# Moving an attention kernel's operands as two parts of 48 rows instead of one of 104

## The chip, the core and the metric

The kernel runs on one core of a Trainium2 chip. The core has five engines with queues of their own: TensorE (PE, with its weight loads as PEld), VectorE (DVE), ScalarE (ACT), GpSimd (POOL) and SyncE (SP), which here issues all transfers and does nothing else. The core's 16 DMA engines carry the transfers. The metric is the device time of one execution in microseconds; a run's result is the median of its executions.

## The reference

Three stages follow each other: a recurrence over 768 steps for 4 x 8 heads of 40 dimensions, a two-layer MLP (320 to 2048 to 320, 3072 tokens) and a mixture of four two-layer experts (320 to 1024 to 320).

```python
for t in range(S):                                    # r, k, v, w, a, b: [4, 8, 768, 40]
    y[:, :, t] = einsum('bhd,bhde->bhe', rt, state)
    Sa = einsum('bhde,bhe->bhd', state, at)
    state = state * wt - outer(Sa, bt) + outer(vt, kt)
x = y as [3072, 320]
x = (h - tanh(h)) @ w_out             with h = x @ w_in
out = sum over e of p[:, e] * (relu(x @ w1[e]) @ w2[e])
```

## The kernel before, in words

**The work.** The 768 steps are cut into 6 chunks of 128. A *unit* is one chunk of a group of four heads (48 units, `i`), and two units make a *pair* (24 pairs, `p`; four pairs make a chunk). Each pair runs on PE as a chain of four blocks of 32 steps, in which PE, DVE and ACT hand small tiles to each other (`right_sides`, `save_right_side`, `answer`, `save_answer`). After the last pair of each chunk from the second on, one pass of the first MLP runs for the chunk before (`mlp`). The experts follow, in a part of the program of their own.

**The operands.** Two heads stand above each other in one tile: rows 0 to 39 and rows 64 to 103. Rows 40 to 63 hold nothing but padding. So every operand tile has 104 rows (`PR = HALF + HD`, 64 + 40). For each unit SP loads raw decays, k, b and a (`raw_parts`, L220) into one of seven buffers at the start and later into one of five and then three (`slot`). DVE scans the decays (L1045) and takes the reciprocal (L1051), POOL scales k and b (L1241) and a (L1244) in place, PE makes the unit's diagonal blocks (`diagonal`, L583), and SP stores the scaled operands to HBM (`store_operands`, L369). For each pair SP later loads them back by pairs of units: k and b (`load_kb`, L379), a (`load_a`, L388) and the decays (`load_decays`, L397).

**The order.** SP's list is written out by hand (`start`, `early_loads`, `pair`, `mlp` of the SP block) and runs strictly in order; each step waits on semaphores for the buffer it writes. A later raw load waits for the store of the unit that had its buffer. During pairs 2 to 7 the same list also brings the first MLP's weights in eight pieces (`raw_piece`, L453: L469, L471 twice, L472), and during pair 5 the first tokens (L449, L451); ACT rounds them (L947 to L949 and L956), POOL takes the rest (L1261 to L1267). ACT does this in line with its other work for the pairs.

**The start.** The loads of the first seven units stand in a program block of their own. All engines leave that block together, when SP has issued the last of its 21 transfers; DVE's first scan comes behind it. From there DVE works through eight units, two masks, two more units and the inverse of the first chunk (L1070 to L1092) before PE can start on pair 0.

Of the kernel before, what the change touches and what calls it, by code (L numbers as in the profile page):

```python
# [26 lines left out]
C = 128  # L27
# [8 lines left out]
HALF = 64  # L36
# [38 lines left out]
def uses(i):  # L75

    return sum(slot(k) == slot(i) for k in range(i + 1))
# [85 lines left out]
def recurrence_and_first_mlp(nc, sem, pairs, ident, kbaw, rvt, vn, w_in, w_out, scratch, turned, middle):  # L163
    ctx = ExitStack()
    with ctx:
# [195 lines left out]
        def _(sp):  # L361
            def load_raw(i):
                j = before(i)
                if j is not None:
                    sp.wait_ge(op_stored[slot(j)], 16 * uses(j))
                    sp.wait_ge(lt_full, j + 1)
                raw_parts(sp, i)

            def store_operands(i):  # L369
                sp.wait_ge(scaled, 2 * (i + 1))  # L370
                sp.dma_start(scratch[i, :, :], raw_of(i)[0:PR, WW:MADE]).then_inc(op_stored[slot(i)], 16)

            def both_units(p):

                for i in (2 * p, 2 * p + 1):
                    sp.wait_ge(op_stored[slot(i)], 16 * uses(i))
                return scratch[2 * p:2 * p + 2, :, :].rearrange("j p w -> p j w")

            def load_kb(p):  # L379

                both = both_units(p)
                if p >= 2:
                    sp.wait_ge(kbn_full[1], p - 1)
                    sp.wait_ge(low_full, p - 1)
                sp.dma_start(kb[:, p % 2, :, :, :, :].rearrange("p j a q t -> p j (a q t)"), both[:, :, 0:OP_A])\
                    .then_inc(kb_in[p % 2], 16)

            def load_a(p):  # L388
# [5 lines left out]
                a = at[:, p % 2, :, :, :].rearrange("p j q t -> p j (q t)")  # L394
                sp.dma_start(a, both[:, :, OP_A:OP_LAM]).then_inc(at_in[p % 2], 16)

            def load_decays(p):  # L397

                both = both_units(p)
                if p >= 2:  # L400
                    sp.wait_ge(y_saved, p - 1)
                    sp.wait_ge(state_ready, p - 1)
                sp.dma_start(lam[:, p % 2, :, :, :].rearrange("p j q t -> p j (q t)"), both[:, :, OP_LAM:OPW])\
                    .then_inc(lam_in[p % 2], 16)

# [47 lines left out]
            def raw_piece(i):  # L453
# [4 lines left out]
                if not earlier:  # L458
                    last = LAST_RAW[piece_slot(i)]
                    sp.wait_ge(op_stored[slot(last)], 16 * uses(last))  # L460
# [108 lines left out]
        def _(pe):  # L569
# [155 lines left out]
            def scores(p, j):  # L725

                if j == 0:
                    pe.wait_ge(kb_in[p % 2], 16 * (p // 2 + 1))
                    pe.wait_ge(at_in[p % 2], 16 * (p // 2 + 1))
                    pe.wait_ge(r_in[p % 3], 64 * (p // 3 + 1))  # L730
# [171 lines left out]
        def _(act):  # L902
# [19 lines left out]
            def save_turned_answers(p):  # L922
                act.wait_ge(ut_full, p + 1)
                if p == 0:
                    act.wait_ge(op_stored[RING + 1], 16)
                act.activation(ut[:, :, :, :].rearrange("p j q t -> p (j q) t"),
                               turn_bank[0:PR, 0:4 * C].rearrange("p (k t) -> p k t", k=4), ACT.Copy).then_inc(ut_saved, 1)
# [108 lines left out]
        def _(dve):  # L1036
# [21 lines left out]
            def inverse(c, first, last):  # L1058
# [4 lines left out]
                for k in range(first, last):  # L1063
                    if k == 0:
# [3 lines left out]
                        elif c:  # L1068
                            dve.wait_ge(op_stored[RING + 1], 16)
                        ins = dve.transpose(lu[:, :, :], ld[:, :, :].rearrange("p h t -> p t h"))  # L1070
# [50 lines left out]
            def mask_ur(p):  # L1121
                dve.wait_ge(ur_full, p + 1)
                if p == 0:
                    dve.wait_ge(op_stored[RING], 16)
                dve.tensor_tensor(out=nu[:, :, :, :, :].rearrange("p s j q t -> p s (j q) t"),
# [13 lines left out]
            def save_result(p):  # L1139
                dve.wait_ge(y_full, p + 1)  # L1140
                dve.wait_ge(lam_in[p % 2], 16 * (p // 2 + 1))
                if p:
# [94 lines left out]
        def _(pool):  # L1237
# [9 lines left out]
            def decay_state(p):  # L1247
                g = 2 * (p % PPC)
                pool.wait_ge(st_read, p + 1)
                pool.wait_ge(lam_in[p % 2], 16 * (p // 2 + 1))  # L1250
                both = st[:, g:g + 2, :, :].rearrange("p j q e -> p (j q) e")
# [307 lines left out]
```

## Time and profile before

| | before |
|---|---|
| median of 3 runs | 1663.45 us (1659.49 to 1669.53) |
| the profiled execution | 1664.84 us, span 1663.1 us |
| PE busy | 1484.1 us, 89% |
| DVE, ACT, POOL busy | 811.2, 420.4, 374.4 us |
| mean granted TensorE clock | 0.953 |
| moved by DMA | 112.84 MB |

The span runs from the first to the last instruction; some 1.7 us of the execution lie around it. Busy time is what an engine spends in instructions; idle time is given to what ended it. Only idle time on the chain that ends last costs anything. SP's rows show how long the issue of a transfer occupied SP's sequencer, not how long the transfer took. The share of DMA is a mean over all 16 engines.

### The profile page before, as it was taken

To read this page: it belongs to the slowest core of one execution; us is meant where nothing else is said; L and a number is where in the kernel's file an instruction comes from. 1 tells how busy PE (TensorE), PEld (TensorE's weight loads), DVE (VectorE), ACT (ScalarE), POOL (GpSimd) and SP (SyncE) were. 2 spreads that over 40 slices of the span, in tenths; PEclk is the share of its full clock that TensorE was granted. 3 is DMA by queue.
4 is the path that set the end of the run, shared out by engine and by line. 5 is a ranking of instruction groups with operands and counts; after the bars stand their busy time and mean duration, and the time that the engine had idled before them with its cause. 6 is when DMAs were issued, how large, how long until landed. Compare 5 with 4: busy or idle time off the path is not lost. (4 is left out here: it accounts for less than half of the span.)

```text
span 1663.1 us, 37883 instructions
## 1 busy us (share of the span) xinstructions
PE 1484.1 (89%) x15888; PEld 1295.1 (78%) x15888; DVE 811.2 (49%) x1396; ACT 420.4 (25%) x859; POOL 374.4 (23%) x314
## 2 busy tenths in 40 slices
PE   2387688998989999999969779999999999999998
PEld 1266566877877877877868679999999999999998
DVE  7959765776865955853211323333333333333333
ACT  1123343343333233333223311111111111111111
POOL 4122553332332322321233340202020202020000
PEclk9978798999998988998989889999999999999999
DMA  6545684065066135111010420101010100000011
GB/s 183 163 129 144 161 216 109 17 179 145 11 161 159 31 109 133 37 56 41 9 35 1 147 70 0 35 0 35 0 35 0 34 0 18 17 0 0 0 47 47
DMA packets 89411, 112.84 MB, mean 68 GB/s; under 512 B 10952, under 2 KB 67400, under 8 KB 89288
## 3 DMA queue, kind: packets, MB, share of 16 engines
q1 hardware_dynamic: 89288, 111.05, 24.2%
q8 instruction: 96, 1.57, 0.4%
q14 instruction: 27, 0.22, 0.0%
HBM read 78.73 MB, written 32.28 MB: 67 GB/s over the span
## 5 line engine op out<-in xcount | busy, mean ns | idle before, releaser
L1443 PE MATMUL banks<-x2t,u 128*128 x1536 | 377.6, 393 | 8.4 <-POOL u L1410 8.4
L1453 PE MATMUL banks<-u,hid 128*128 128x320 f32 x2304 | 360.6, 309 | 0.0
L1453 PEld LDWEIGHTS banks<-u,hid 128*128 128x128 f32 x2304 | 349.0, 188 | 11.2
L1508 DVE SCALAR_TENSOR_TENSOR hid<-banks,hid 128x512 fp32r<-128x512 f32 x192 | 132.7, 691 | 414.0 <-ACT hid L1478 414.0
L1443 PEld LDWEIGHTS banks<-x2t,u 128*128 128x128 f32 x1536 | 284.2, 189 | 61.3 <-issue 8.6
L1478 ACT ACTIVATE hid<-banks 128x512 fp32r<-128x512 f32 x192 | 115.0, 599 | 581.5 <-PE banks L1443 581.5
L859 PE MATMUL banks<-xt,wi 128*128 128x512 f32 x768 | 197.6, 400 | 20.5 <-issue 12.8
L868 PE MATMUL banks<-wo,hid 128*128 128x320 f32 x1152 | 183.8, 309 | 5.6 <-POOL hid L1283 5.6
L868 PEld LDWEIGHTS banks<-wo,hid 128*128 128x128 f32 x1152 | 175.4, 188 | 14.1 <-POOL hid L1283 6.4
L859 PEld LDWEIGHTS banks<-xt,wi 128*128 128x128 f32 x768 | 142.3, 191 | 48.4 <-issue 13.9
L1283 POOL TENSOR_TENSOR hid<-shared,hid 128x512 fp32r<-128x512 f32 x96 | 123.5, 1287 | 226.8 <-ACT hid L1011 226.5
L1209 DVE TENSOR_TENSOR shared<-banks,shared 128x512 f32<-128x512 f32 x96 | 66.1, 688 | 140.5 <-ACT shared L1004 140.3
L1515 DVE SCALAR_TENSOR_TENSOR acc<-banks,pn,acc 128x320 f32 x192 | 92.5, 544 | 60.4 <-PE banks L1453 60.4
L1004 ACT ACTIVATE shared<-banks 128x512 f32<-128x512 f32 x96 | 57.5, 599 | 238.8 <-PE banks L859 237.4
L1402 POOL CAST u<-raw 128x1024 fp32r<-128x1024 f32 x8 | 8.3, 1041 | 475.8 <-PE banks L1453 455.7
L913 ACT ACTIVATE un<-banks 32x160 f32<-32x160 f32 x192 | 56.5, 294 | 207.2 <-PE banks L629 204.8
L1108 DVE TENSOR_TENSOR rhs<-banks,own 128x160 f32<-128x160 f32 x192 | 52.9, 316 | 110.3 <-PE banks L619 105.5
L1241 POOL TENSOR_TENSOR made<-made 104x512 f32<-104x512 f32 x41 | 52.1, 1270 | 231.9 <-DVE made L1051 231.9
L629 PE MATMUL banks<-rhs,tt 128*32 128x160 f32 x384 | 55.9, 359 | 41.9 <-DVE rhs L1108 40.8
L1083 DVE TENSOR_TENSOR ld<-ld,tmp 128x31 f32<-128x31 f32 (+15 forms) x186 | 89.4, 481 | 5.2
L1086 DVE TENSOR_TENSOR tmp<-tt,ld 128x31 f32<-128x31 f32 (+15 forms) x155 | 73.0, 471 | 4.5
L1134 DVE TENSOR_TENSOR nvmak<-banks,upper 128x1024 f32<-128x1024 f32 x48 | 58.5, 1218 | 32.3 <-PE banks L746 32.3
(112 smaller groups left out, 1553.3 us busy)
## 6 DMA issues: line engine op xcount, KB each, us to landing
scaled_operands<-made SPq DMA_DIRECT2D x41, 416.8 KB
made<-kbaw SPq DMA_DIRECT2D x41, 312.0 KB
kb<-scaled_operands SPq DMA_DIRECT2D x24, 416.0 KB
raw<-w SPq DMA_DIRECT2D x8, 640.0 KB, 5.6
lam<-scaled_operands SPq DMA_DIRECT2D x24, 209.6 KB
at<-scaled_operands SPq DMA_DIRECT2D x24, 208.0 KB
raw<-w SPq DMA_DIRECT2D x8, 512.0 KB, 4.0
rt<-rvt SPq DMA_DIRECT2D x96, 40.0 KB
```

Source lines behind the costliest of these rows:

```text
L859: mm = pe.matmul(solve_bank(f % 2), wi[:, w, part], xt[:, x, :], start=(n == 0), stop=(n == 7))
L868: mm = pe.matmul(down_bank[t][:, 0:D], hid[:, f % HIDS, h, part], wo[:, w, f, :], start=(f == 0 and n == 0), stop=(f == NF1 - 1 and n == 2))
L1083: ins = dve.tensor_tensor(out=ti[:, j + 1:, 0:ncol], in0=ti[:, j + 1:, 0:ncol], in1=t, op=ALU.subtract)
L1086: ins = dve.tensor_tensor(out=t, in0=bc(lu[:, j + 1:, j:j + 1], [128, nr, ncol]), in1=bc(ti[:, j:j + 1, 0:ncol], [128, nr, ncol]), op=ALU. ...
L1134: dve.tensor_tensor(out=nvmak[:, j, :, :, :, :].rearrange("p s a q t -> p s (a q) t"), in0=score_pair[:, :, :].rearrange("p s (k t) -> p s ...
L1209: dve.tensor_tensor(out=gap[:, f % 2, :], in0=solve_bank(f % 2), in1=gap[:, f % 2, :], op=ALU.subtract)\
L1283: pool.tensor_tensor(out=hid[:, f % HIDS, 1, :], in0=gap[:, f % 2, :], in1=hid[:, f % HIDS, 0, :].bitcast(F32), op=ALU.subtract).then_inc( ...
L1443: mm = pe.matmul(p_up[f][:], u1[:, par, w, f * 128:(f + 1) * 128], xt[:, x, cols], start=(i == 0), stop=(i == 7))
L1453: mm = pe.matmul(p_dn[t][:, 0:D], hid[:, f, h, t * 128:(t + 1) * 128], u2[:, par, w, f, :], start=(f == 0 and i == 0), stop=(f == NFU - 1 ...
L1478: act.activation(hid[:, f, 0, :], p_up[f][:], ACT.Relu).then_inc(e_hi, 1)
L1508: dve.scalar_tensor_tensor(out=hid[:, f, 1, :], in0=p_up[f][:], scalar=0.0, in1=hid[:, f, 0, :].bitcast(F32), op0=ALU.max, op1=ALU.subtract)\
L1515: dve.scalar_tensor_tensor(out=a, in0=p_dn[t][:, 0:D], scalar=pn[:, bass.ds(n * BATCH + t, 1), bass.ds(e, 1)] .rearrange("p o e -> p (o e) ...
```

## The change

Every transfer of 104 rows becomes two of 48, and the rows 48 to 55, which are padding, are left out. Where a buffer or a place in HBM is used for the first time, the upper part has 56 rows instead (0 to 55), so that the padding is filled once: for the raw loads of units 0 to 6, the stores of units 0 to 3 and the loads of pairs 0 and 1. The raw load had three transfers per unit and keeps three, cut in another way: the a operand, which stands at another column for the lower head, now comes with the rest for the upper rows. The store of a unit and the three loads of a pair had one transfer each and have two; the semaphores they count on are waited for at 32 instead of 16.

```diff
+ROWS = 48
         def raw_parts(eng, i):
             to, a = raw_of(i), WW + OP_A
-            eng.dma_start(to[0:PR, 0:a], kbaw[i, :, 0:a]).then_inc(raw_op_in[slot(i)], 16)
-            eng.dma_start(to[0:HALF, a:a + 2 * C], kbaw[i, 0:HALF, a:a + 2 * C]).then_inc(raw_op_in[slot(i)], 16)
-            eng.dma_start(to[HALF:PR, a:a + 2 * C], kbaw[i, HALF:PR, a + 2 * C:a + 4 * C]).then_inc(raw_op_in[slot(i)], 16)
+            top, bottom = row_parts(before(i) is None)
+            eng.dma_start(to[top, 0:a + 2 * C], kbaw[i, top, 0:a + 2 * C]).then_inc(raw_op_in[slot(i)], 16)
+            eng.dma_start(to[bottom, 0:a], kbaw[i, bottom, 0:a]).then_inc(raw_op_in[slot(i)], 16)
+            eng.dma_start(to[bottom, a:a + 2 * C], kbaw[i, bottom, a + 2 * C:a + 4 * C]).then_inc(raw_op_in[slot(i)], 16)
+
+        def row_parts(filled):
+            return slice(0, PR - ROWS if filled else ROWS), slice(PR - ROWS, PR)
...
             def store_operands(i):
                 sp.wait_ge(scaled, 2 * (i + 1))
-                sp.dma_start(scratch[i, :, :], raw_of(i)[0:PR, WW:MADE]).then_inc(op_stored[slot(i)], 16)
+                for part in row_parts(i < 4):
+                    sp.dma_start(scratch[i, part, :], raw_of(i)[part, WW:MADE]).then_inc(op_stored[slot(i)], 16)
...
-                sp.dma_start(kb[:, p % 2, :, :, :, :].rearrange("p j a q t -> p j (a q t)"), both[:, :, 0:OP_A])\
-                    .then_inc(kb_in[p % 2], 16)
+                for part in row_parts(p < 2):
+                    sp.dma_start(kb[part, p % 2, :, :, :, :].rearrange("p j a q t -> p j (a q t)"), both[part, :, 0:OP_A])\
+                        .then_inc(kb_in[p % 2], 16)
```

`load_a` and `load_decays` are changed as `load_kb` is, and every wait on `op_stored`, `kb_in`, `at_in` and `lam_in` counts by 32.

What SP issues in its first block, in program order: before, each unit has three rows, the first of 104 rows by 768 words, into the buffers `made`, `spare` and `shared` from the input `kbaw`.

```order
1 L223 DMA made<-kbaw 104x768
2 L224 DMA made<-kbaw 64x256
3 L225 DMA made<-kbaw 40x256
4 L223 DMA made<-kbaw 104x768
5 L224 DMA made<-kbaw 64x256
```

And now, at the same place:

```order
1 L225 DMA made<-kbaw 56x1024
2 L226 DMA made<-kbaw 48x768
3 L227 DMA made<-kbaw 48x256
4 L225 DMA made<-kbaw 56x1024
5 L226 DMA made<-kbaw 48x768
```

The number of transfers in the block stays at 21; their shapes are new.

SP's list in pair 5, from the store of a unit's scaled operands over the first tokens and a piece of the weights to the load of a, before:

```order
167 L371 DMA scaled_operands<-made 104x1026 [waits operands_scaled]
168 L439 DMA tokens_turned<-shared 40x4x128 [waits result_saved]
169 L439 DMA tokens_turned<-shared 40x4x128
170 L403 DMA lam<-scaled_operands 104x2x258 [waits result_saved,state_ready,operands_stored1,operands_stored0]
171 L449 DMA spare<-tokens_turned 128x2x512 [waits weight_lo_split,tokens_stored]
172 L451 DMA spare<-tokens_turned 64x512 x2
173 L469 DMA spare<-w_in 128x2x256 [waits weight_lo_split]
174 L471 DMA spare<-w_in 64x256 x2
175 L472 DMA spare<-w_out 128x2x320
176 L395 DMA at<-scaled_operands 104x2x256 [waits right_side_full0,right_side_full1,operands_stored3,operands_stored2]
```

And the list now, some rows further on, in the part between the load of a and the next load of the decays, where the store, the loads of k and b (`kb`), a (`at`) and the decays (`lam`) each have a second row:

```order
221 L403 DMA at<-scaled_operands 48x2x256 [waits right_side_full0,right_side_full1,operands_stored3,operands_stored2]
222 L403 DMA at<-scaled_operands 48x2x256
226 L393 DMA kb<-scaled_operands 48x2x512 [waits natural_full1,low_scores_full,operands_stored1,operands_stored0]
227 L393 DMA kb<-scaled_operands 48x2x512
228 L378 DMA scaled_operands<-made 48x1026 [waits operands_scaled]
229 L378 DMA scaled_operands<-made 48x1026
230 L225 DMA made<-kbaw 48x1024 [waits diagonal_full,operands_stored1]
231 L226 DMA made<-kbaw 48x768
232 L227 DMA made<-kbaw 48x256
242 L413 DMA lam<-scaled_operands 48x2x258 [waits result_saved,state_ready,operands_stored3,operands_stored2]
243 L413 DMA lam<-scaled_operands 48x2x258
```

No step changes its place and no wait is added; five transfers per pair are. No other engine has an instruction more or less.

## Rows read from the trace of the kernel before

**Rows 1.** The page: the span of the profiled execution.
```profile
span 1663.1 us, 37883 instructions
```

**Rows 2.** Windows by stage: length, each engine's busy time, PEclk, DMA share, GB/s.
```profile
11.70:76.00 64.30, 15.75 (x444) 13.22 (x444) 60.69 (x103) 7.15 (x18) 19.98 (x20) 1.00 0.64 176
163.00:262.00 99.00, 70.94 (x1668) 57.14 (x1665) 63.11 (x101) 40.72 (x95) 47.91 (x44) 0.83 0.74 194
362.00:379.00 17.00, 15.46 (x416) 12.47 (x416) 12.39 (x21) 8.16 (x21) 8.50 (x8) 1.00 0.71 187
937.00:1663.00 726.00, 705.60 (x3984) 639.05 (x3984) 240.22 (x406) 125.05 (x210) 81.32 (x49) 0.98 0.08 27
```

**Rows 3.** Timeline of the start: start us, us, engine, line, operation, idle before and releaser.
```profile
2.50 0.34 SPq L223 DMA_DIRECT2D made<-kbaw  x1
2.88 0.48 SPq L224 DMA_DIRECT2D made<-kbaw  x1
3.40 0.51 SPq L225 DMA_DIRECT2D made<-kbaw  x1
...
10.62 0.51 SPq L225 DMA_DIRECT2D shared<-kbaw  x1
...
11.70 0.74 DVE L1045 TENSOR_TENSOR_SCAN made<-made 104x128 f32<-104x128 f32 x2 [7.80 <-PEq L274]
...
74.78 0.62 PE L629 MATMUL banks<-rhs,tt 128*32 128x160 f32 x2 [24.73 <-DVE rhs L1108]
```

**Rows 4.** Timeline of SP: issues that stand behind another issue, and one that does not.
```profile
94.48 0.30 SPq L371 DMA_DIRECT2D scaled_operands<-made  x1
...
213.47 0.59 SPq L469 DMA_DIRECT2D spare<-w_in  x1
...
214.10 0.47 SPq L471 DMA_DIRECT2D spare<-w_in  x1
...
214.62 0.60 SPq L471 DMA_DIRECT2D spare<-w_in  x1
```

**Rows 5.** Windows with transfers of 104 rows, with transfers of 128, and around unit 15.
```profile
60.00:62.00 2.00, 0.00 (x0) 0.00 (x0) 1.83 (x6) 0.00 (x0) 0.00 (x0) 1.00 0.80 227
...
333.00:335.00 2.00, 1.90 (x54) 1.48 (x43) 2.00 (x4) 0.52 (x2) 0.82 (x1) 1.00 1.00 341
...
95.00:105.00 10.00, 7.38 (x197) 5.59 (x193) 3.40 (x5) 2.25 (x7) 2.79 (x3) 0.50 0.83 214
```

**Rows 6.** Timeline around unit 15's raw load, all engines.
```profile
97.51 0.52 SPq L225 DMA_DIRECT2D spare<-kbaw  x1
...
104.75 0.74 DVE L1045 TENSOR_TENSOR_SCAN spare<-spare 104x128 f32<-104x128 f32 x2 [5.43 <-DMA spare<-kbaw]
...
105.65 0.47 PE L583 MATMUL banks<-made 40*32 40x32 f32 x17 [2.31 <-issue]
...
108.06 0.75 PE L629 MATMUL banks<-rhs,tt 128*32 128x160 f32 x4
```

**Rows 7.** Waits of ACT from 50 to 330 us: in total, times, longest.
```profile
ACT wi L947 <- DMA spare<-w_out: 5.0, 5, 1.5
ACT xt L956 <- DMA spare<-tokens_turned: 1.1, 1, 1.1
```

**Rows 8.** Waits of PE from 76 to 262 us.
```profile
PE banks L583 <- ACT ld L908: 5.6, 3, 3.0
...
PE banks L583 <- issue: 2.3, 1, 2.3
```

**Rows 9.** Waits of PE from 250 to 280 us.
```profile
PE banks L859 <- POOL wo L1267: 7.7, 1, 7.7
```

**Rows 10.** Waits of SP from 163 to 262 us.
```profile
SPq L223 <- DMA scaled_operands<-made: 6.9, 3, 3.0
SPq L371 <- POOL made L1244: 6.4, 5, 3.1
```

**Rows 11.** Waits of SP from 330 to 937 us.
```profile
SPq L422 <- PE banks L746: 30.0, 12, 2.9
```

More of the change, by code:

```diff
@@ L364, in load_raw @@
                 if j is not None:
-                    sp.wait_ge(op_stored[slot(j)], 16 * uses(j))
+                    sp.wait_ge(op_stored[slot(j)], 32 * uses(j))
                     sp.wait_ge(lt_full, j + 1)
@@ L393, in load_a @@
                         sp.wait_ge(sma_full[j], NB * (p - 1))
-                a = at[:, p % 2, :, :, :].rearrange("p j q t -> p j (q t)")
-                sp.dma_start(a, both[:, :, OP_A:OP_LAM]).then_inc(at_in[p % 2], 16)
+                for part in row_parts(p < 2):
+                    sp.dma_start(at[part, p % 2, :, :, :].rearrange("p j q t -> p j (q t)"), both[part, :, OP_A:OP_LAM])\
+                        .then_inc(at_in[p % 2], 16)
             def load_decays(p):
@@ L402, in load_decays @@
                     sp.wait_ge(state_ready, p - 1)
-                sp.dma_start(lam[:, p % 2, :, :, :].rearrange("p j q t -> p j (q t)"), both[:, :, OP_LAM:OPW])\
-                    .then_inc(lam_in[p % 2], 16)
+                for part in row_parts(p < 2):
+                    sp.dma_start(lam[part, p % 2, :, :, :].rearrange("p j q t -> p j (q t)"), both[part, :, OP_LAM:OPW])\
+                        .then_inc(lam_in[p % 2], 16)
             def turned_input(p, which):
@@ L459, in raw_piece @@
                     last = LAST_RAW[piece_slot(i)]
-                    sp.wait_ge(op_stored[slot(last)], 16 * uses(last))
+                    sp.wait_ge(op_stored[slot(last)], 32 * uses(last))
                     sp.wait_ge(lt_full, last + 1)
@@ L727, in scores @@
                 if j == 0:
-                    pe.wait_ge(kb_in[p % 2], 16 * (p // 2 + 1))
-                    pe.wait_ge(at_in[p % 2], 16 * (p // 2 + 1))
+                    pe.wait_ge(kb_in[p % 2], 32 * (p // 2 + 1))
+                    pe.wait_ge(at_in[p % 2], 32 * (p // 2 + 1))
                     pe.wait_ge(r_in[p % 3], 64 * (p // 3 + 1))
@@ L924, in save_turned_answers @@
                 if p == 0:
-                    act.wait_ge(op_stored[RING + 1], 16)
+                    act.wait_ge(op_stored[RING + 1], 32)
                 act.activation(ut[:, :, :, :].rearrange("p j q t -> p (j q) t"),
@@ L1068, in inverse @@
                         elif c:
[L1069 removed]
+                            dve.wait_ge(op_stored[RING + 1], 32)
                         ins = dve.transpose(lu[:, :, :], ld[:, :, :].rearrange("p h t -> p t h"))
@@ L1123, in mask_ur @@
                 if p == 0:
-                    dve.wait_ge(op_stored[RING], 16)
+                    dve.wait_ge(op_stored[RING], 32)
                 dve.tensor_tensor(out=nu[:, :, :, :, :].rearrange("p s j q t -> p s (j q) t"),
@@ L1140, in save_result @@
                 dve.wait_ge(y_full, p + 1)
-                dve.wait_ge(lam_in[p % 2], 16 * (p // 2 + 1))
+                dve.wait_ge(lam_in[p % 2], 32 * (p // 2 + 1))
                 if p:
@@ L1249, in decay_state @@
                 pool.wait_ge(st_read, p + 1)
-                pool.wait_ge(lam_in[p % 2], 16 * (p // 2 + 1))
+                pool.wait_ge(lam_in[p % 2], 32 * (p // 2 + 1))
                 both = st[:, g:g + 2, :, :].rearrange("p j q e -> p (j q) e")
```

2 lines of the change are left out of this document (1 added, 1 removed).

## The prediction

> **What bounds the kernel now.** I read the page's span first [rows 1] and then cut it into stages with windows. The reader is to see which engine is full in each [rows 2]. From 937 us to the end (the experts) PE is busy 705.6 of 726 us, and the DMA share is 0.08. No operand of this change moves there, so 726 us cannot change. From 11.7 to 76 us DVE is busy 60.69 of 64.3 us. It works through scans, reciprocals and the inverse while PE waits for it: the first answer of pair 0 starts at 74.78 us after an idle time of 24.73 us that DVE ended [rows 3]. What delays DVE in this stage delays everything behind it. A later pair, such as the one from 362 to 379 us, takes 17 us, of which PE works 15.46 [rows 2], and what DMA brings is no part of PE's waits there. Only from 76 to 262 us does the pair stage have holes; from 163 to 262 us PE works 70.94 of 99 us, and the DMA share of 0.74 is the highest of the long stages.
>
> Next I asked the waits who waits for a transfer. DVE waits once, 5.43 us, for the raw load of unit 15 [rows 6]. ACT waits five times, 5.0 us in all, for weight pieces, and once, 1.1 us, for the tokens [rows 7]. That is 11.5 us, all between 95 and 262 us. It is the most that quicker operand transfers can return by direct waits, if each of these waits lies on the path. Last I read SP's own queue, since the change gives SP more to issue: 48 stores (one per unit) and 3 x 24 loads (k and b, a, decays per pair) become two each, 120 issues more; the raw loads stay at three per unit.
>
> **The start.** DVE's first scan waits for the end of the program block, and that is the end of SP's 21st issue: SP ends at 10.62 + 0.51 = 11.13 us, and DVE starts at 11.70 [rows 3]. DVE is full from there, so a change in the sum of these issues goes onto the path one to one. The transfers themselves are not what it waits for at this point, since the wait is ended by the block.
>
> One unit takes 0.34 + 0.48 + 0.51 = 1.33 us of issue before [rows 3]. The new shapes are not in the trace. Issues range from 0.30 us for one with nothing just ahead of it to 0.60 us for a load of 64 rows behind another such load [rows 4]. From below, three times 0.30 makes 0.90 us per unit, a gain of 0.43 x 7 = 3.0 us. From above, I take the three rows of a weight piece in the places of the new three: 0.59 behind a 64-row load, then 0.47 and 0.60, which makes 1.66 us and a loss of 0.33 x 7 = 2.3 us. The new loads are two-dimensional, stand behind each other and fill part of a row, as the 64-row loads do, so the value is near the upper end: **+1.8 us**.
>
> **How much quicker the transfers are.** Where only raw loads and a store of 104 rows are in flight, the share of the 16 engines stays at 0.80, at 227 GB/s; with 128- and 64-row loads of the tokens it is 1.00, at 341 GB/s [rows 5]. So the 104-row transfers seem to leave about a fifth of the engines without work. Bytes fall to 96/104, or 0.923. If the engines without work get their part too, a burst of such transfers takes 0.923 x 0.80 = 0.74 of its time; if not, 0.923. The two ends are a cut of 26% and one of 8%. I take the first, as the share at 128 rows is the nearest row on even loads.
>
> The Trainium skill (DMA: Bandwidth & Descriptors, section "Why a DMA increments its semaphore by 16 and not by 1") says that a transfer is spread over the largest number of engines, up to 16, that divides its slowest dimension. By that rule the trace agrees: it gives 13 engines for 104 rows, 0.81 of 16, and 16 for 48. The same page (section "Rules for kernel authors") speaks against the change: two transfers to separate parts of the partitions run one behind the other on the same engines, and one transfer is to be used. By that sentence alone the sum would hold the cost of the issues and the 8% of bytes, and nothing else.
>
> **Unit 15.** Its last part is issued at 97.51 us, DVE's scan starts at 104.75 [rows 6], and the ten microseconds before it run at a share of 0.83 [rows 5]. A cut of 26% on some 8 us of backlog is 2.1 us, a cut of 8% is 0.6 us. Against it stand one more store issue and a dearer raw load ahead of it, 0.3 to 0.6 and 0.3 us. DVE's wait falls by 1.3 us at best guess. What PE gains is less. PE stops in the middle of a group of diagonal blocks, until 105.65 us, with 2.31 us of idle time that no operand ended ("issue"), and then runs the scores of the next pair up to the answer at 108.06 [rows 6]. The right side that DVE wrote was ready by then. What hides DVE's gain is PE's own gap; with the gap gone, the full 2.1 us would count. I book **-0.5 us**, between 0 and -4.4 (2.1 and the gap of 2.31 [rows 8]).
>
> **Weight pieces.** ACT waits 6.1 us in all [rows 7]. Behind three of these waits, PE waits for ACT's copy of a diagonal block, 5.6 us in all [rows 8]. Weight and token loads have 128 and 64 rows and stay as they are; they gain only by what runs beside them. They are issued behind the store and the decays of the same pair, two more issues of 0.30 to 0.60 us. So each of the four or five pieces comes 0.6 to 1.2 us later by its issue, and earlier by some 0.7 to 1.5 us of a backlog of some 6 us, of which operands are roughly half (26% of 3 us is 0.8). That is near zero; I book **-0.5 us**, from -4 to +4. The last piece ends in PE's wait of 7.7 us for POOL at the first MLP [rows 9]. Nearly all of that is ACT's and POOL's work behind the transfer, and it stays.
>
> **The later pairs.** Each pair gets five issues more, 1.5 to 3.0 us, and two raw loads that are dearer by 0.33 us each: up to 3.7 us of SP per pair. Behind an issue that comes late on SP stand the loads of v and natural v, k and b of the pair after next, and the next store. In these pairs SP waits for others: 12 times for the scores, 30.0 us, before it may load v [rows 11]. At 2.5 us each that is most of the added issues, and a shorter backlog also frees SP sooner from its waits on stores. I book 0. What covers it is the time between the load of v and the scores of the pair after, about half a pair, 8 us; it costs up to 3.7 us per pair once SP's list takes longer than the 17 us of a pair.
>
> **The sum.** Against the profiled execution: 1664.84 (the span of 1663.1 and 1.7 around it) + 1.8 - 0.5 - 0.5 = 1665.6 us. That execution lay 1.4 us above the median of the runs, 1663.45, so the median should come to about **1664 us**. The runs before lie 10 us apart, 0.6%; a change within 0.5% (8.3 us) can hardly be told from none, and this forecast is inside.
>
> **The rivals.** *Faster: DMA is the hidden bound of pairs 1 to 7.* If every wait there that a transfer starts goes away, together with PE's gap, it is 5.4 + 5.6 + 2.3 = 13.3 us; if the start costs nothing as well, 1663.5 - 13.3 = 1650 us, and with three quarters of it about 1653. For it speaks the DMA share of 0.74 and the 0.80 that looks like a ceiling. Against it: DVE's 5.4 us is mostly covered by PE's own order, and pieces wait for issues too. *Slower: SP's queue becomes the bound where the weights are loaded.* From 163 to 262 us SP waits only 6.4 us for POOL and 6.9 us for its own stores [rows 10], over five pairs; the issues added are 5 x 3.7 = 18.5 us. The point from which it decides is a share of DMA that does not rise, so that landings shrink by 8% only: then pieces, raws and k and b come later in each of five pairs by 1.5 to 3 us, in all 7 to 15 us, and 2.3 at the start: 1673 to 1681, about 1676 us. *The change doesn't do what it says:* the share stays at 0.80, the issues cost what they cost, and SP still has room: 1663.5 + 2 = 1665.5, which the measurement can't tell from the forecast.
>
> **How the numbers follow.** The forecast has 0.55 and no relief with room on SP 0.20, both within 0.5%. The faster rival has 0.12 and the slower one 0.13. Of these two a few cases end inside, and the first two let a few out by the spread of the runs. Faster by over 0.5% is 0.13, within 0.5% 0.74, slower 0.13. The likeliest case has 1658 to 1670 (bounds -3.0 to +2.3, 0 to -4.4, -4 to +4, not all at one side). For 8 in 10 I reach halfway to both rivals: 1654 to 1673.
>
> **What would show it.** Right: DVE's first scan at 12.5 to 14 us instead of 11.70; the share of DMA near 1.0 where raw loads and stores run alone (60 to 62 us); DVE's wait for unit 15 at 3 to 5 us; ACT's waits for pieces between 4 and 8 us; pairs of 17 us as before; SP's wait for the scores down from 30.0 us. Wrong: new waits of PE at L746 or of POOL for the decays, a pair of over 17.5 us, or a first scan before 11 us. The granted clock is a thing that I can't steer: it was 0.50, the lower level of 1.2 GHz, from 95 to 105 us [rows 5], in a stretch in which PE worked 7.38 of 10 us and had stood idle for 24.73 us some time before [rows 3], and a shift of its stretches by itself moves a few us.

## The result, and the profile after

The changed kernel takes **1651.99 us** (median of 10 runs, 1646.25 to 1656.90) beside 1661.32 us for the kernel before (10 runs, 1655.46 to 1669.85): a ratio of **0.9935, 95% interval 0.9911 to 0.9959**. The forecast was 1664 and the range ended at 1654, so the time is 2 us below the range. A second measurement gave 0.9959 (0.9929 to 0.9989). The gain is 0.4 to 0.65%, at the edge of what I had called measurable.

The page of the changed kernel: span, busy time by engine, and the DMA queues.
```profile
span 1650.1 us, 38003 instructions
...
PE 1481.8 (90%) x15888; PEld 1293.5 (78%) x15888; DVE 812.0 (49%) x1396; ACT 420.6 (25%) x859; POOL 374.9 (23%) x314
...
q1 hardware_dynamic: 87542, 106.83, 24.0%
q8 instruction: 96, 1.57, 0.4%
```
The windows that answer to [rows 2] and [rows 5], with the same columns. The fourth ends with the span as its partner does, so it starts some 12 us later in the program.
```profile
11.70:76.00 64.30, 16.89 (x457) 14.00 (x461) 60.73 (x101) 6.17 (x19) 19.99 (x20) 1.00 0.64 171
163.00:262.00 99.00, 72.85 (x1635) 58.48 (x1636) 59.57 (x95) 37.01 (x89) 48.38 (x44) 0.79 0.69 177
362.00:379.00 17.00, 15.53 (x422) 12.52 (x418) 12.51 (x21) 6.63 (x17) 6.25 (x7) 1.00 0.71 187
937.00:1650.00 713.00, 700.50 (x3953) 634.71 (x3952) 235.33 (x399) 122.80 (x206) 74.93 (x48) 0.99 0.07 23
...
60.00:62.00 2.00, 0.00 (x0) 0.00 (x0) 1.86 (x5) 0.00 (x0) 0.00 (x0) 1.00 0.96 267
95.00:105.00 10.00, 8.23 (x203) 6.13 (x201) 5.71 (x10) 2.11 (x7) 2.94 (x4) 0.67 0.69 157
```
From 60 to 62 us, where only operands of this change are in flight, the share is 0.96 where it was 0.80 [rows 5], at 267 GB/s for 227: the transfers are quicker, as forecast. In the long stage from 163 to 262 us the share is 0.69 for 0.74 [rows 2].

The timeline of the start, which answers to [rows 3].
```profile
2.19 0.41 SPq L225 DMA_DIRECT2D made<-kbaw  x1
2.64 0.36 SPq L226 DMA_DIRECT2D made<-kbaw  x1
3.05 0.42 SPq L227 DMA_DIRECT2D made<-kbaw  x1
...
9.66 0.42 SPq L227 DMA_DIRECT2D shared<-kbaw  x1
...
10.53 0.74 DVE L1055 TENSOR_TENSOR_SCAN made<-made 104x128 f32<-104x128 f32 x2 [6.62 <-PEq L280]
...
73.64 0.62 PE L639 MATMUL banks<-rhs,tt 128*32 128x160 f32 x2 [24.76 <-DVE rhs L1118]
```
The three issues of a unit take 0.41 + 0.36 + 0.42 = 1.19 us, not 1.33 [rows 3], and not the 1.59 of my forecast. The block ends earlier, the first scan starts at 10.53 us instead of 11.70, and PE's first answer at 73.64 instead of 74.78 [rows 3].

Unit 15 and the answer of PE behind it, which answer to [rows 6].
```profile
96.54 0.46 SPq L227 DMA_DIRECT2D spare<-kbaw  x1
...
101.55 0.74 DVE L1055 TENSOR_TENSOR_SCAN spare<-spare 104x128 f32<-104x128 f32 x2 [4.25 <-DMA spare<-kbaw]
...
104.31 0.83 PE L639 MATMUL banks<-rhs,tt 128*32 128x160 f32 x4 [1.68 <-DVE rhs L1118]
```
DVE waits 4.25 us for the raw load instead of 5.43, and the 2.31 us in which PE stood still without a releaser [rows 6] are not here. In the two repeats of the changed kernel, below, this wait of DVE was 5.85 and 4.83 us, and the stop was back.

The waits that answer to [rows 7], [rows 8], [rows 9], [rows 10] and [rows 11]: of ACT from 50 to 330 us, of PE from 76 to 262 us, of SP from 163 to 262 us and from 330 to 937 us.
```profile
ACT wi L957 <- DMA spare<-w_out: 2.9, 2, 2.3
```
```profile
PE banks L869 <- POOL wo L1277: 7.3, 1, 7.3
...
PE banks L593 <- ACT ld L918: 4.7, 2, 3.2
```
```profile
SPq L378 <- POOL made L1254: 6.9, 4, 3.2
SPq L225 <- DMA scaled_operands<-made: 3.1, 2, 2.2
```
```profile
SPq L432 <- PE banks L756: 16.6, 11, 2.3
```
All but one are shorter: SP's wait for POOL went from 6.4 [rows 10] to 6.9. But direct waits for data account for little: ACT's 6.1 us [rows 7] fell to 2.9, PE's behind ACT from 5.6 [rows 8] to 4.7, PE's for the last weight piece from 7.7 [rows 9] to 7.3. What is larger is a kind of idle time of PE that I had seen once in the trace of before and not looked for elsewhere. These are the stops of PE between 330 and 860 us, of at least 0.7 us, that nothing in the profile ended, first in the timeline of the kernel before,
```profile
387.48 0.20 PE L606 MATMUL banks<-vnat,nvmak 128*32 128x40 f32 x1 [2.71 <-issue]
...
467.26 0.27 PE L742 MATMUL banks<-rt,vt 40*128 40x128 f32 x1 [0.92 <-issue]
...
500.14 0.35 PE L629 MATMUL banks<-rhs,tt 128*32 128x160 f32 x1 [1.07 <-issue]
...
519.91 0.21 PE L583 MATMUL banks<-made 40*32 40x32 f32 x1 [1.13 <-issue]
...
604.79 0.23 PE L606 MATMUL banks<-vnat,nvmak 128*32 128x40 f32 x2 [1.08 <-issue]
```
and then in the timeline of the changed kernel, which has no others from 76 us on either.
```profile
459.46 0.27 PE L752 MATMUL banks<-rt,vt 40*128 40x128 f32 x1 [0.91 <-issue]
...
591.45 0.23 PE L616 MATMUL banks<-vnat,nvmak 128*32 128x40 f32 x2 [0.81 <-issue]
```
The kernel before has one more, earlier, besides the 2.31 us at 105.65 [rows 6].
```profile
98.38 0.48 PE L619 MATMUL banks<-un,low 96*32 96x40 f32 x12 [0.97 <-issue]
```
So before has 10.2 us of such stops from 76 to 860 us, the changed kernel 1.7. From its first matmul with the experts' weights (L1443 before, L1453 now) to the start of its last, the expert stage takes 691.1 us before and 690.4 now. (One pause of PE of 12.4 to 13.1 us in the first MLP, L859 before and L869 now, has no releaser either; it is in all profiles and left out.)

### The profile page after: what moved, and what is told of

It is laid out like the page before. It is cut to its first block and busy times, and to the rows that moved or that the text cites. A ratio compares the mean times of both kernels' runs of the same rounds, so it can differ in the third digit from the quotient of the medians.

```text
span 1650.1 us, 38003 instructions
## 1 busy us (share of the span) xinstructions
PE 1481.8 (90%) x15888; PEld 1293.5 (78%) x15888; DVE 812.0 (49%) x1396; ACT 420.6 (25%) x859; POOL 374.9 (23%) x314
## 2 busy tenths in 40 slices
DMA packets 87666, 108.63 MB, mean 66 GB/s; under 512 B 13630, under 2 KB 66686, under 8 KB 87542
## 5 line engine op out<-in xcount | busy, mean ns | idle before, releaser
L1453 PE MATMUL banks<-x2t,u 128*128 x1536 | 376.9, 392 | 7.9 <-POOL u L1420 7.9
L1453 PEld LDWEIGHTS banks<-x2t,u 128*128 128x128 f32 x1536 | 283.7, 189 | 60.8 <-issue 8.2
L869 PE MATMUL banks<-xt,wi 128*128 128x512 f32 x768 | 196.8, 399 | 19.8 <-issue 12.6
L869 PEld LDWEIGHTS banks<-xt,wi 128*128 128x128 f32 x768 | 141.8, 191 | 47.6 <-issue 13.6
L639 PE MATMUL banks<-rhs,tt 128*32 128x160 f32 x384 | 55.9, 358 | 42.6 <-DVE rhs L1118 42.5
```

Of the source, the lines that this page charges most:

```text
L869: mm = pe.matmul(solve_bank(f % 2), wi[:, w, part], xt[:, x, :], start=(n == 0), stop=(n == 7))
L1453: mm = pe.matmul(p_up[f][:], u1[:, par, w, f * 128:(f + 1) * 128], xt[:, x, cols], start=(i == 0), stop=(i == 7))
```

## The experiments

Each ratio is to the kernel before on the same chip, with its 95% interval. It is the ratio on record for all comparable executions, and it can lie up to 0.2% from the quotient of the two medians. Single executions of one kernel lie up to 1.5% apart here (1651.49 to 1676.50 us), so the ratio decides, and a profile only shows places.

### Three repeats: what one profile is worth

The two kernels were run again unchanged.

> The kernel before once more, unchanged, for a second profile: which of TensorE's stops without a releaser (at 98.4, 105.7, 387.5, 467.3, 500.1, 519.9 and 604.8 us, 10.2 us together) and of the half-clock stretches come again. Theory F (they belong to the load on the DMA engines): at least five of the seven come again within 2 us of their place in the program. Rival N (they fall by chance from one execution to the next): two or fewer.

> The changed kernel once more, unchanged, for a second profile. Theory F: again no stop over 0.9 us without a releaser but that at 459 us. Rival N: some of those of before show here.

> The changed kernel unchanged, timed on the same chip as the next three. 0.991 to 0.996 of before.

The changed kernel timed once more gave 1651.12 us beside 1660.57 (medians): 0.9959 (0.9929 to 0.9989). The stops of at least 0.7 us in the second execution of before:
```profile
98.40 0.48 PE L619 MATMUL banks<-un,low 96*32 96x40 f32 x12 [0.92 <-issue]
...
105.95 0.47 PE L583 MATMUL banks<-made 40*32 40x32 f32 x17 [2.58 <-issue]
...
231.35 0.29 PE L606 MATMUL banks<-vnat,nvmak 128*32 128x40 f32 x4 [1.10 <-issue]
...
374.20 0.43 PE L629 MATMUL banks<-rhs,tt 128*32 128x160 f32 x2 [0.79 <-issue]
...
470.78 0.27 PE L742 MATMUL banks<-rt,vt 40*128 40x128 f32 x1 [1.11 <-issue]
...
518.79 0.21 PE L583 MATMUL banks<-made 40*32 40x32 f32 x1 [0.77 <-issue]
...
637.96 0.24 PE L606 MATMUL banks<-vnat,nvmak 128*32 128x40 f32 x3 [1.20 <-issue]
```
and in the second execution of the changed kernel:
```profile
102.38 0.34 PE L593 MATMUL banks<-made 40*32 40x32 f32 x17 [3.28 <-issue]
...
206.96 0.49 PE L756 MATMUL banks<-at,kb 40*128 40x128 f32 x4 [0.79 <-issue]
...
465.65 0.27 PE L752 MATMUL banks<-rt,vt 40*128 40x128 f32 x1 [1.14 <-issue]
...
596.07 0.23 PE L616 MATMUL banks<-vnat,nvmak 128*32 128x40 f32 x2 [0.84 <-issue]
```
Of the seven stops of before, four come again near their place in the program (98, 106, 471 and, at 0.77 us, 519 us), which lies between the two theories (five or more, two or fewer). For the changed kernel the rival came true: the stop at unit 15 is there, at 3.28 us. In the third execution it is the only one, of 2.22 us. So whether a stop comes at one of its places differs from one execution to the next, and the reader must not take 10.2 against 1.7 us for the size of the effect.

What five executions together give, in us (PE's waits are the rows that the view of PE's waits lists over the span, added up by releaser; its "issue" includes the pause, 12.6 to 12.9 us in these five):

| execution | span | PE busy | waits: issue | POOL | ACT | DVE |
|---|---|---|---|---|---|---|
| before | 1663.1 | 1484.1 | 23.4 | 55.9 | 21.8 | 60.2 |
| before, second | 1659.5 | 1482.4 | 22.1 | 56.1 | 21.3 | 59.4 |
| changed | 1650.1 | 1481.8 | 14.5 | 53.9 | 20.2 | 61.8 |
| changed, second | 1654.4 | 1482.0 | 19.6 | 54.3 | 19.0 | 61.0 |
| changed, third | 1647.8 | 1476.9 | 16.6 | 55.0 | 19.9 | 60.8 |

From the mean of the two to the mean of the three the span falls by 10.5 us: 5.9 in the stops without a releaser, 3.0 in PE's busy time for the same 15,888 matmuls (its clock), 1.9 in waits for ACT, 1.6 for POOL, and DVE gives 1.4 back. These add up to 11.0; gaps too short for the list give 0.5 back. Over half of this difference is thus in the stops, but it is a difference of five profiles: the two of before have 10.2 and 8.5 us of stops over 0.7 us, the three of the changed kernel 1.7, 6.1 and 2.2.

Where the time goes can be read from the start of one and the same matmul, found by its place in PE's order (counted from 0; the order is the same in all kernels but for a few neighbours), in us:

| matmul | before | before, second | changed | second | third | change of the mean |
|---|---|---|---|---|---|---|
| 408, first answer of pair 0 | 74.78 | 74.85 | 73.64 | 73.64 | 73.58 | -1.2 |
| the answer behind unit 15 [rows 6] | 108.06 | 108.36 | 104.31 | 105.30 | 104.20 | -3.6 |
| 4408, in pair 8 | 345.23 | 349.00 | 341.38 | 346.64 | 340.34 | -4.3 |
| 8911, a later pair | 639.99 | 634.67 | 624.29 | 627.60 | 625.82 | -11.4 |
| 12048, first with the experts' weights | 966.86 | 963.04 | 954.57 | 957.86 | 951.70 | -10.2 |

About 1 us of the difference is at the start, 3 us between there and 345 us, and 7 us in the pairs from 345 to 640 us; the experts add nothing. The two executions of before lie up to 5.3 us apart in this table, so each share is good to a few us only.

### Which transfers carry it

Raw loads alone in the new form:
```diff
 # kernel before; stores and loads of scaled operands untouched
-            eng.dma_start(to[0:PR, 0:a], kbaw[i, :, 0:a])...
+            top, bottom = row_parts(before(i) is None)
+            eng.dma_start(to[top, 0:a + 2 * C], kbaw[i, top, 0:a + 2 * C])...
 # and the other two transfers of the unit, as in the change
```


> The kernel before with the change made in the raw loads alone (its three transfers per unit cut in the new way); stores and loads of the scaled operands stay at 104 rows. Theory 1 (even load): raw loads are a third of the operand bytes; the first scan comes 1.2 us sooner, unit 15's load a little, and some of PE's unexplained idle times stay: 1655 to 1659 us. If the start and the shape of the raw loads are all that counts, it is the changed kernel's 1650 to 1654. If the relief comes from stores and loads of scaled operands alone, 1660.

Measured: 0.9989 (0.9964 to 1.0015).

Scaled operands alone, twice, on two chips (the changed kernel with `raw_parts` of before):

> Stores and loads of the scaled operands in two parts of 48 rows; all raw loads as before. With the raw loads alone in the new form the time was 1660.4 against 1658.6 of before, so if the parts add up, nearly all of the gain is here: 1651 to 1655 us. Rival (the gain needs both, because it comes from the total load on the DMA engines falling under what the instruction fetches can live with): 1655 to 1658 us.

> Stores and loads of scaled operands in two parts of 48, raw loads as before, once more on the chip of the other two. The same 0.9937 as in the first run if that was right (0.991 to 0.997).

Measured: 0.9937 (0.9908 to 0.9967) and 0.9963 (0.9938 to 0.9987), the gain of the whole change.

Of the scaled operands, the loads alone in two parts of 48 rows:
```diff
 def store_operands(i):
-                for part in row_parts(i < 4):
+                for part in (slice(0, PR),):
 # and 16 for 32 in the waits on op_stored; raw loads as before
```


> Only the loads of scaled operands (kb, at, lam) in two parts of 48 rows; the stores and the raw loads as before. If the loads carry the gain, 0.993 to 0.996 of before. If the stores carry it (SyncE waits for them to land before it can issue the loads), 0.998 to 1.000.

Measured: 1.0015 (0.9987 to 1.0043): nothing. The stores alone, and then all but the stores:
```diff
 # kernel before
-                sp.dma_start(scratch[i, :, :], raw_of(i)[0:PR, WW:MADE])...
+                for part in (slice(0, 56), slice(56, PR)):
+                    sp.dma_start(scratch[i, part, :], raw_of(i)[part, WW:MADE])...
 # changed kernel
-                for part in row_parts(i < 4):
+                for part in (slice(0, PR),):
```


> The kernel before with only the stores of scaled operands in two parts, of 56 and 48 rows (all rows, since the loads still read all of them). Theory W (a store in two parts lands earlier; SyncE and the next raw load into the slot wait for it): 0.994 to 0.997 of before. Theory L (load on the DMA engines as a whole): bytes are as before, 0.998 to 1.001.

> The changed kernel with the stores of scaled operands in one transfer of 104 rows as before. Theory W: the gain is gone, 0.998 to 1.001 of before. Theory L: about two thirds of the gain stay, since raw loads and loads of scaled operands still move fewer rows, 0.995 to 0.998.

Measured: 0.9973 (0.9939 to 1.0007) and 0.9974 (0.9948 to 0.9999). Each point is about half of the gain, but neither interval parts the two theories. That the stores are needed for the whole gain is supported by three runs (loads alone nothing, loads and stores all, all but the stores half); that they are enough is not shown. The mechanism that I had named for it falls, though. SP's wait for a store before the next raw load into its slot, over the whole span, in the loads-alone kernel and in the one with all but the stores:
```profile
SPq L224 <- DMA scaled_operands<-made: 18.1, 10, 4.4
```
```profile
SPq L225 <- DMA scaled_operands<-made: 23.6, 12, 5.3
```
The same wait in the kernel before, and in the changed one:
```profile
SPq L223 <- DMA scaled_operands<-made: 28.7, 13, 6.7
```
```profile
SPq L225 <- DMA scaled_operands<-made: 14.1, 7, 3.3
```
The loads alone take away 10.6 of it and the time does not move. So this wait of SP decides nothing.

### Where in the program

Three kernels use the new form for a part of the units only: all but the raw loads of the first seven, units 0 to 15 (pairs 0 to 7), and units 16 to 47.
```diff
+            if before(i) is None:       # first kernel: units 0 to 6, loads as before
...
+def in_two(i):
+    return i < 16          # second kernel; in the third: i >= 16
...
+            if not in_two(i):
+                eng.dma_start(to[0:PR, 0:a], kbaw[i, :, 0:a])...
...
-            return slice(0, PR - ROWS if filled else ROWS), slice(PR - ROWS, PR)
+            if i is not None and not in_two(i):
+                return (slice(0, PR),)
```


> The changed kernel, with the raw loads of the first seven units (those that the start issues) in the form of before. It tells where the start's 1.17 us came from. Theory S (SyncE issues the three transfers of a unit in 1.19 us instead of 1.33, so the seventh unit lands earlier): the first scan moves back from 10.53 to about 11.7 us of the span, the whole is 1 to 1.5 us slower than the changed kernel, 1653 to 1654 us. Theory B (the load per engine of the first burst): the first scan moves back as well, but SyncE's last issue of the burst does not, it stays at 9.66. If the start is worth nothing to the end, the time stays at 1652.

> The new form for units 0 to 15 (pairs 0 to 7: their raw loads, stores, and loads of scaled operands), the old one for units 16 to 31. Theory D (the gain lies where data are awaited directly: the start, unit 15, the weight pieces, all before 345 us): the whole gain, 1650 to 1654 us. Theory F (the gain is in TensorE's stops that nothing in the profile ends, with the half-clock stretches behind them, which in the profile of before lay at 98, 105 and also at 387, 467, 500, 519 and 604 us): about half, 1654 to 1657 us.

> The new form for units 16 to 31 (pairs 8 to 15) alone; the start and pairs 0 to 7 are as before. Theory D (direct waits before 345 us): no gain, 1658 to 1661 us. Theory F (stops of TensorE and half-clock stretches behind them, anywhere): about half of the gain, 1653 to 1657 us.

With the old first loads: 0.9955 (0.9931 to 0.9980), first scan back at 11.68 us and SP's 21st issue back at 10.62. So the start's 1.17 us is the form of those seven units and SP's issues of them; whether it comes through to the end, 0.07%, is below what these intervals can tell. The first pairs alone gave 0.9985 (0.9955 to 1.0015), the later ones alone 0.9970 (0.9943 to 0.9997). A gain that lies only before 345 us, in direct waits, would have given the whole to the first and none to the second. The points speak against it, but the first interval reaches to 0.9955 and the second to 0.9997, so it is not excluded. (The texts of the last two expectations speak of units 16 to 31; they stand for all units from 16 on.)

### Rows, spread, and parts

All of these move everything in two parts; they differ in the rows.
```diff
-            return slice(0, PR - ROWS if filled else ROWS), slice(PR - ROWS, PR)
+            return slice(0, PR // 2), slice(PR // 2, PR)                 # 52 + 52
+            return slice(0, PR - ROWS), slice(PR - ROWS, PR)             # 56 + 48
+            return slice(0, HALF if filled else HD), slice(HALF, PR)     # 40 + 40
+            return slice(0, PR - n if filled else n), slice(PR - n, PR)  # n = 40 or 32, raw 48 or 40
```


> The changed kernel with parts of 52 and 52 rows: two issues where it has two, but every one of the 104 rows is moved. Theory 1 (even load): the 104-row transfers kept the share of the 16 DMA engines at 0.80, and what the change brought is that the busiest engines have less to carry, so that raw loads, weight pieces and PE's own instructions come sooner. The Trainium skill's rule for the number of engines (DMA: Bandwidth & Descriptors) gives 13 for 52 rows as for 104. If that is so, this kernel keeps the share near 0.80 in 60 to 62 us, keeps idle times of PE that nothing in the profile ended (7 of 0.9 us or more from 76 to 620 us before, 9.3 us in all), and comes at 1658 to 1663 us against 1661 before. Theory 2 (fewer bytes): no bytes are left out, so no gain either, 1660 to 1663. Theory 3 (two transfers in flight instead of one, and cheaper issues at the start): most of the gain is here, 1650 to 1655.

> The changed kernel with the upper part at 56 rows always, so that all 104 rows move. Theory 1 (even load): the busiest engine carries 4 + 3 = 7 rows of a tile (by the Trainium skill's rule 56 rows go to 14 engines and 48 to 16) against 8 before and 6 in the change; about half of the gain or more, 1653 to 1658 us. Theory 2 (fewer bytes): none are left out, so only the start's 1.2 us, 1660 us. Theory 3: as the changed kernel, 1650 to 1655.

> The changed kernel with parts of 40 and 40 rows (64 and 40 at a first use): all 24 rows of padding are left out, 80 of 104 rows move. Theory 1 (even load): by the Trainium skill's rule for the number of engines a part of 40 rows is on 10 engines, 4 rows each, so the busiest carry 8 rows of a tile as they did for 104 rows; the gain is that of the start alone, 1658 to 1662 us, the DMA share stays under 0.7 where operands move alone, and PE's unexplained idle times stay. Theory 2 (fewer bytes): 23% fewer operand bytes against 8% in the change, so it is faster than the changed kernel, 1640 to 1650 us. Theory 3 (two transfers instead of one): as the changed kernel, 1650 to 1655.

> Raw loads in two parts of 48 rows as in the changed kernel, scaled operands in two parts of 40. Theory L: 16 rows less of each scaled operand than in the changed kernel, 0.989 to 0.992 of before. If 40 rows lose in spread over the engines what they save in bytes, as two parts of 40 for all operands did, 0.993 to 0.995.

> Raw loads in two parts of 40 rows, stores and loads of scaled operands in two parts of 32 rows (they leave out eight rows of each half that hold data, so that the answer's rows 32 to 39 of each half are of old data). Bytes and DMA load fall once more by as much as from the kernel before to two parts of 40. If the gain goes by the load on the DMA engines, 1644 to 1648 us; if what could be had from the load is already had with 48 or 40 rows, 1649 to 1652 us.

| rows (scaled operands) | time, us | ratio, interval | stops of PE over 0.7 us |
|---|---|---|---|
| 52 + 52 | 1657.07 | 0.9990 (0.9971 to 1.0009) | 3.0 |
| 56 + 48 | 1653.89 | 0.9974 (0.9951 to 0.9996) | 4.4 |
| 48 + 48 (the change, two measurements) | 1651.99, 1651.12 | 0.9935, 0.9959 | 1.7, 6.1, 2.2 |
| 40 + 40 | 1650.16 | 0.9931 (0.9906 to 0.9957) | 2.2 |
| 40 + 40, raw 48 + 48 | 1651.26 | 0.9938 (0.9910 to 0.9966) | 3.3 |
| 32 + 32, raw 40 + 40 | 1643.64 | 0.9879 (0.9835 to 0.9923) | 0.8 |

Two parts as such gain nothing that can be measured (52 + 52). The same bytes spread more evenly (56 + 48) gain perhaps a quarter of a per cent; the two intervals overlap. Fewer rows gain, and the last row of the table, whose kernel leaves out eight rows with data of each half of the scaled operands, shows that it goes on below 80 rows. Its chip had the slowest kernel before of all (1666.76 us), and one execution of the changed kernel on it took 1656.06 us. Between 96 and 80 rows nothing is seen. Of those that move all rows with data, none is measurably better than the change.

No theory of these expectations holds alone. Even load had 1658 to 1662 us for 40 + 40, where 1650.16 was measured, and it had PE's stops stay with 52 + 52 and 40 + 40, where they are 3.0 and 2.2 us. Bytes alone had a gain from 96 to 80 rows.

The Trainium skill (DMA: Bandwidth & Descriptors, section "Why a DMA increments its semaphore by 16 and not by 1") spreads a transfer over the largest number of engines, up to 16, that divides its rows: 13 for 104 and for 52, 16 for 48, 10 for 40. The traces agree: from 40 to 66 us the commonest number of packets in flight at once, other than none, is 13 in both executions of before and with 52 + 52, 10 with 40 + 40, and 15 or 16 in the three of the changed kernel. For 56 rows the rule gives 14. The times of 52 + 52 and 56 + 48 agree with it, if weakly; that of 40 + 40 shows that the spread alone does not decide. The advice of the same page (section "Rules for kernel authors") against two transfers to separate partitions agrees with 52 + 52 (0.9990) and not with 48 + 48, where a part spreads over more engines than the whole did and idle rows are left out.

### Is it the load as such?

The changed kernel with a copy that nothing waits for:
```diff
+                sp.dma_start(idle[i, :, :], kbaw[i, 0:ROWS, 0:OPW]).then_inc(idle_done, 16)
```


> The changed kernel with one more transfer for each of the 48 units, that nothing waits for: 48 rows of raw input are copied from HBM to a tensor in HBM that is not read. The bytes moved rise by about 9 MB read and 9 MB written. Theory L (what counts is the load on the DMA engines): the gain is gone and more, 1.000 to 1.010 of before. Rival O (what counts is how soon the kernel's own transfers land, by their own rows and engines): most of the gain stays, 0.994 to 0.998.

Measured: 1658.34 us, 0.9981 (0.9955 to 1.0008), beside 0.9959 for the changed kernel on the same chip. The page counts 118.09 MB for 108.63. About half of the gain seems gone, between the two expectations, though the intervals of 0.9981 and 0.9959 overlap. What it costs is not in the stops. The stops of this kernel are one:
```profile
465.97 0.37 PE L755 MATMUL banks<-rt,vt 40*128 40x128 f32 x1 [1.17 <-issue]
```
and its waits of PE for the first answers and the last weight piece, over the span,
```profile
PE banks L642 <- DVE rhs L1121: 43.9, 14, 24.7
...
PE banks L872 <- POOL wo L1280: 9.9, 1, 9.9
```
were 41.5 and 8.0 us in the changed kernel profiled with it (42.5 and 7.3, 41.7 and 7.3 in the other two). In this one profile the added bytes come back as some 4 us of direct waits, not as stops.

## Why the prediction was wrong

**What bounds the kernel**: right as to stages. The expert stage did not change, and the stretch from 362 to 379 us has the same busy times; DVE's first scan moved what is behind it one to one up to the first answer (1.17 and 1.14 us). But "what DMA brings is no part of PE's waits there" was read from waits with a releaser only.

**The start** had the wrong sign: +1.8 forecast, -1.2 measured. The failed step is "so the value is near the upper end". I took a weight load's 0.47 to 0.60 for the new loads because they are two-dimensional; they cost 0.36 to 0.42. In the trace of before, the row of the same tensor that was nearest in kind, the load of the first columns at 0.34 [rows 3], was the better measure; the lower bound of -3.0 did hold the value. A first scan before 11 us, which came (10.53), stood among the signs of being wrong.

**Quicker transfers** was right: share 0.96 for a forecast of near 1.0.

**Unit 15** and **the weight pieces** had the sign right and were booked too small. DVE's wait fell by 1.2 us in the first profiles (forecast 1.3), but that is luck: in all five it is 5.43 and 5.45 us before, 4.25, 5.85 and 4.83 after, a fall of 0.5 in the mean, while DVE is 1.2 us ahead from the start. PE's answer behind unit 15 came 2.4 us sooner beyond the start's 1.2, for 0.5 booked, inside the bound of 4.4; PE's own gap did not go, it is in two of the three changed executions. ACT's waits for pieces and tokens fell to 2.9 us, below the 4 to 8 named as the sign. Over the span, PE's waits for ACT and POOL together fell by 3.5 us in the mean, for the 1.0 us booked on the two steps.

**The later pairs** is the step that put the number outside the range: "I book 0", with a loss of up to 3.7 us per pair as the only other case. From 345 to 640 us the mean of the executions fell by 7 us. SP's queue had room, as the text says (its wait for the scores went from 30.0 [rows 11] to 16.6 us), but a gain was given no chance there. PE's stops without a releaser, of which the gap at unit 15 [rows 6] was one, fell by 5.9 us over the span in the mean, and its busy time by 3.0. Another 2.1 us of the miss is no step's: the forecast started from a median of three runs, 1663.45 us, and that of ten is 1661.32.

**The rivals.** The faster one, "DMA is the hidden bound of pairs 1 to 7", had 0.12 and 1650 to 1653 us, which is the time, by luck: its place was wrong in the main, as units 0 to 15 alone gave 0.9985 and the later ones 0.9970. The slower one, SP's queue, is refuted: with 120 issues more the kernel is faster. PE waits for a transfer once in either kernel, 10.7 us before the experts. Only DVE's short waits for raw loads other than unit 15's grew, from 0.2 and 1.6 us to 2.1, 3.3 and 1.4.

**What the stops belong to.** Over all 20 profiles of this study, add up PE's stops of at least 0.7 us from 76 to 860 us. In the ten executions in which some transfers of raw or scaled operands still go as 104 rows beyond the first seven units, they come to 3.5 to 10.2 us, 6.9 in the mean (before 10.2 and 8.5; raw loads alone 6.8; scaled alone 6.3 and 5.9; pairs 0 to 7 7.5; later pairs 7.7; loads alone 7.8; stores alone 3.5; all but the stores 5.0). In the ten in which none does, 0.8 to 6.1 us, 2.7 in the mean (the changed kernel 1.7, 6.1 and 2.2; old first loads 2.3; 52 + 52 3.0; 40 + 40 2.2; 56 + 48 4.4; 48 and 40 3.3; 32 0.8; idle copies 1.2). Nine of ten lie above 4.9 on one side, nine of ten below 4.5 on the other. So single transfers of 104 rows go with the stops, and added bytes do not. This is a sorting of profiles after the fact, not an experiment made for it, and the time does not follow the stops alone: 52 + 52 and the idle copies have few and little gain, while the scaled operands alone have the whole gain with 6.3 and 5.9 us of stops. PE's busy time for the same matmuls differs more, from 1473.9 to 1494.0 us over the 20 profiles.

What the stops are can be read from the packets in the traces. In a stop PE mostly stands in the middle of a group of matmuls and waits for nothing that the profile shows. The page has a queue of 96 packets of 16 KB that are instructions, and in all 20 traces these start at nearly the same places of PE's order, one per about 127 matmuls. Of the 67 stops, 62 end 1.28 to 1.74 us after such a packet has ended; moments that lie so make up 5% of the time from 76 to 860 us. So nearly all stops end with a block of instructions. In the 14 stops of over 2 us the packet took 1.0 to 1.8 us (the mean of all is 1.1) but began late, from 0.9 us before PE stood still to 1.3 us after. The Trainium skill (Runtime: NRT & Kernel Launch, section "Instruction fetch mechanics") says that a sequencer fetches its instructions in such blocks over a DMA queue of its own, and that this is mostly hidden; the traces agree on both, with 1 to 7 stops for 88 or 89 packets from 76 to 860 us. What makes a block late, and how the rows of other transfers bear on it, no run here shows. What stays open besides is what ties the remaining 3 to 5 us, the clock's share above all, to the transfers.

## What to carry to other kernels

Before giving a price of zero to a stage, add up PE's idle time without a releaser over the whole span, and in two profiles, since here it held 5.9 of the 10.5 us between the profiles and each instance came and went from one execution to the next. Look where the packets of the instruction queue lie beside it. The number of rows of a transfer matters by how it spreads and by how many rows it leaves out; cutting it in two as such gained nothing measurable here, and cost nothing where the queue that issues it had waits to spend. For the price of an issue take the row of the same tensor and a like shape, not that of a load of other shape in another place.

## What was unexpected of the hardware

- Three issues on SP of the new raw loads took 1.19 us, those of before 1.33, although the first of the new ones has rows of 4 KB, where the longest of before have 3 KB (a load of 312 KB in 104 rows): the length of the rows did not set the cost. With 64 and 40 rows in the 40 + 40 kernel the second unit's three took 0.49 + 0.51 + 0.33 = 1.33 us, with 52 and 52 rows 3 x 0.37 = 1.11, and the first scans came at 11.62 and 10.09 us.
- Of 67 stops of PE without a releaser, 62 ended 1.28 to 1.74 us behind a packet of the instruction queue.
- PE stood still 0.7 to 4.0 us, with no releaser in the profile, at places that recur across kernels: 26 of the 67 stops lie at 97 to 108 us, 18 at 456 to 477, 7 at 371 to 396, 5 at 635 to 642, 4 at 591 to 607, and 7 elsewhere; each execution has some of them.
- Behind such a stop the granted clock was at the lower level of 1.2 GHz in the first profile of before, though it was also there at 388 us in the second, which has no stop at 387. Here are two stretches of the first,
```profile
388.00:391.00 3.00, 3.00 (x28) 2.29 (x30) 1.63 (x5) 0.58 (x2) 0.00 (x0) 0.54 0.75 201
501.00:507.00 6.00, 6.00 (x92) 4.87 (x90) 1.80 (x5) 0.58 (x2) 1.07 (x2) 0.50 0.62 168
```
  and the same of the second execution.
```profile
388.00:391.00 3.00, 3.00 (x52) 2.30 (x46) 2.22 (x3) 0.92 (x4) 0.27 (x1) 0.50 0.67 183
501.00:507.00 6.00, 5.82 (x171) 4.61 (x160) 4.11 (x8) 1.65 (x6) 4.33 (x4) 1.00 0.75 195
```
  The 6 us from 501 us hold 92 matmuls in the one and 171 in the other. Which stretches fall to the lower level differs between two executions of one kernel.
